# LayerNorm's output transposed by VectorE and DMA instead of TensorE, in a kernel of attention and an MLP

## The reference

```python
q_rot, k_rot = rotate(q), rotate(k)
scores = (1 / sqrt(64)) * q_rot @ k_rot.T
attn = exp(scores - max(scores)); attn = attn / (sum(attn) + 1e-9)
x = (attn @ v), heads side by side                  # 2304 x 512
h = x @ w_in                                        # 2304 x 1024
e = exp(h - max(h)); sm = e / (sum(e) + 1e-9)
solu = h * sm
ln = (solu - mean(solu)) / sqrt(var(solu) + 1e-6) * g_ln
out = ln @ w_out                                    # 2304 x 512
```

## Time and profile before

| | |
|---|---|
| Median of 3 runs | 521.86 us (521.09 to 523.84) |
| The profiled execution | 523.28 us, of which the span 521.5 us |
| TensorE busy | 495.7 us, 95% |
| VectorE busy | 341.9 us, 66% |
| ScalarE busy | 253.5 us, 49% |
| GpSimd busy | 117.3 us, 22% |
| DMA, mean | 84 GB/s; 27.7% of the 16 engines' time |
| Mean granted clock of TensorE | 0.993 |

### The profile page before, as it was taken

The page is one execution under the profiler, slowest core; times in us unless marked ns, Lnnn a source line. Parts: engine busy times, 40 slices in busy tenths (PEclk is TensorE's granted clock), DMA queues, the critical chain, the costliest instruction groups (busy, mean ns, idle before and its releaser), DMA issues.

```text
span 521.5 us, 7337 instructions
## 1 busy us (share of the span) xinstructions
PE 495.7 (95%) x2608; PEld 413.9 (79%) x2608; DVE 341.9 (66%) x554; ACT 253.5 (49%) x379; POOL 117.3 (22%) x84
## 2 busy tenths in 40 slices
PE   0799999989999999999999998999999999999997
PEld 0578888878888888888888876888888888888876
DVE  6957766776777677767774257967555666666550
ACT  3356776766677767776784341322222222222121
POOL 4701254235423542354321101001000000000000
PEclk9799999999999999999999999999999999999999
DMA  9115344534454545453612210010100000000001
GB/s 295 47 27 140 125 150 114 151 124 142 133 146 143 159 105 150 144 163 93 172 30 75 67 43 24 1 64 20 41 20 21 20 22 21 21 20 21 20 35 47
DMA packets 42789, 43.77 MB, mean 84 GB/s; under 512 B 31617, under 2 KB 31617, under 8 KB 40833
## 3 DMA queue, kind: packets, MB, share of 16 engines
q1 hardware_dynamic: 42728, 43.30, 27.7%
q10 hardware_dynamic: 24, 0.00, 0.0%
HBM read 33.63 MB, written 4.79 MB: 74 GB/s over the span
## 4 chain that ended last, share of the span: by engine, by line
PE 80%; issue 5%; SPq 5%; DMA 4%; DVE 3%; ACT 2%; ACTq 0%; POOL 0%; DVEq 0%; POOLq 0%
PE ps L831 19%; PE ps L858 18%; PE ps L844 17%; PE ps L800 14%; PE ps L773 7%; PE ps L868 3%; DMA w_raw<-w_in 3%; PE ps L813 2%; SPq L225 1%; DMA X<-x_in 1%; DVE nm L581 1%; SPq L216 1%; ACT p_main L434 1%; SPq L255 0%; SPq L254 0%
## 5 line engine op out<-in xcount | busy, mean ns | idle before, releaser
L581 DVE TENSOR_REDUCE nm<-ps 128x1 fp32r<-128x576 f32 x144 | 108.5, 756 | 74.9 <-PE ps L773 73.0
L831 PE MATMUL ps<-p_main,V 128*128 128x288 f32 x512 | 146.2, 409 | 0.0
L434 ACT ACTIVATE p_main<-ps 128x576 f32<-128x576 f32 x128 | 83.0, 648 | 52.8 <-PE ps L800 50.9
L800 PE MATMUL ps<-QK 128*128 128x288 f32 x320 | 97.4, 386 | 6.8 <-ACT p_main L434 3.7
L831 PEld LDWEIGHTS ps<-p_main,V 128*128 128x128 f32 x512 | 91.2, 192 | 14.3 <-ACT p_main L434 0.2
L858 PE MATMUL ps<-w_hi,QK 128*128 128x512 f32 x288 | 101.7, 421 | 0.0
L844 PE MATMUL ps<-w_hi,KB 128*128 128x512 f32 x288 | 92.8, 393 | 0.0
L773 PE MATMUL ps<-QK 128*128 128x288 f32 x320 | 68.8, 309 | 13.8 <-ACT QK L408 12.3
L800 PEld LDWEIGHTS ps<-QK 128*128 128x128 f32 x320 | 58.6, 192 | 27.6 <-ACT p_main L434 8.3
L317 POOL TENSOR_TENSOR X<-X,rope 128x1152 f32<-128x1152 f32 x14 | 37.1, 2653 | 141.3 <-DVE w_lo L598 112.0
L800 PE MATMUL ps<-KB 128*128 128x288 f32 x320 | 68.7, 297 | 0.0
(11 more groups left out here) (66 smaller groups left out, 523.8 us busy)
## 6 DMA issues: line engine op xcount, KB each, us to landing
X<-x_in SPq DMA_DIRECT2D x14, 1152.0 KB, 5.1
V<-v_in SPq DMA_DIRECT2D x32, 160.0 KB, 2.8
out<-X SPq DMA_DIRECT2D x18, 256.0 KB, 2.0
w_raw<-w_in SPq DMA_DIRECT2D x16, 256.0 KB, 3.0
xT<-oe SPq DMA_DIRECT2D x16, 144.0 KB, 2.4
inv<-inv_rows SPq DMA_DIRECT2D x16, 144.0 KB, 3.0
xT<-oe SPq DMA_DIRECT2D x16, 128.0 KB, 2.3
inv<-inv_rows SPq DMA_DIRECT2D x16, 128.0 KB, 3.0
```

What stands on the lines that cost most here:

```text
L434: nc.scalar.activation(dst[:, :].rearrange("p (b c) -> p b c", b=2), score_ps[:, :, 0:HALF], ACT.Exp, scale=SCALE).then_inc(exp_done, 1)
L581: nc.vector.tensor_reduce(nm[g][:, at:at + 1], src[:, :, 0:HALF], AX_XY, ALU.max, negate=True)\
L800: ins = nc.tensor.matmul(score_ps[:, half, 0:HALF], keys[:, of:of + P], queries[:, to + half * HALF:to + (half + 1) * HALF], start=(g == 0 ...
L831: ins = nc.tensor.matmul(o_ps[a][:, half, 0:HALF], v, p[:, half * HALF:(half + 1) * HALF], start=(k == 0), stop=(k == 9))
```

## The change

LayerNorm's output is no longer transposed by TensorE. VectorE transposes `ln` in 32 by 32 blocks in place (`turn_l`, one instruction of 128x1024), SP moves the 12 groups of blocks that belong to other partitions by DMA (`move_l`; each DMA has 32 partitions of 8 pieces of 128 bytes), GpSimd copies the 4 that stay (`stay`). `ln_high` and `ln_low` then read SBUF instead of PSUM. The buffers are the old `oe` and `V` of attention. The banks that are free so hold a third h; ups run four tiles ahead instead of three, with up(0) in steps 0 to 2 of the last pair, ups 1 to 3 after attention, and ups 16 and 17 back to back after down(12). SP issues move_l(t+3) after the store of tile t; moves 0, 1 and 2 stand between the last sums, output moves and inverses of attention.

At attention's start: the loads of pair 0 are merged into three; two memsets and the copies of the second queries of pair 0 go to GpSimd; TensorE multiplies the identity (24 times before the first row scores, once after each, 8 times before the first scores); the maxima of pair 1 are spread otherwise over the steps of pair 0, the first four in two PSUM slots. `w_raw` gets a second buffer. The order of the four parts of x in memory changes, so that one multiply by the table of cosines and sines serves keys and one queries.

```diff
-FIRST_MAXIMA = [[], [], [], [0], [1, 2], [3, 4], [5, 6], [7], [8]]
+FIRST_MAXIMA = [([], []), ([], []), ([], [0]), ([1], [2]), ([3], [4]), ([5], []), ([6], []), ([7], []), ([8], [])]
+SPARE = 4
+WARM_START, WARM_ROW, WARM_SCORE = 24, 1, 8
...
-        w_raw = sb("w_raw", [P, 512])
+        w_raw = [sb(f"w_raw{c}", [P, 512]) for c in range(2)]
...
-        h_ps = [ps[:, 0:2, :], ps[:, 2:4, :]]
-        t_ps = ps[:, 4:6, :]
+        h_ps = [ps[:, 0:2, :], ps[:, 2:4, :], ps[:, 4:6, :]]
+        turned_l = [oe[a][:, :, :].rearrange("p a s -> p (a s)")[:, 0:FF] for a in range(2)]
+        ln_T = [V[a][:, :, :, :].rearrange("p a b d -> p (a b d)")[:, 0:FF] for a in range(2)]
...
+        def blocks(l, group, k):
+            part = l[group * TURN:(group + 1) * TURN, :]
+            return part.rearrange("p (c k b) -> p c k b", k=GROUPS, b=TURN)[:, :, k, :]
+        def max_slot(k):
+            if k < STEPS:
+                return max_ps[k % 3], k - 2
+            if k < STEPS + SPARE:
+                return max_ps[2 * ((k - STEPS) % 2)], k - 1
+            return max_ps[0], k
+        def later(t):
+            last = TILES - 1 - AHEAD
+            return [] if t >= last else [t + AHEAD, t + AHEAD + 1] if t == last - 1 else [t + AHEAD]
...
+            def move_l(t):
+                a = t % 2
+                sp.wait_ge(l_turned, t + 1)
+                if t < 2:
+                    sp.wait_ge(pv_done, PVS * (PAIRS - 1 + t))
+                else:
+                    sp.wait_ge(l_lo_done, t - 1)
+                for of in range(GROUPS):
+                    for to in range(GROUPS):
+                        if of != to:
+                            sp.dma_start(blocks(ln_T[a], to, of), blocks(turned_l[a], of, to)).then_inc(l_moved[a], 16)
...
-            load_w(PAIRS - 1)
+            move_l(0)
             inverse_out(PAIRS - 2)
             sums(PAIRS - 1)
             move_o(PAIRS - 1)
             inverse_in(PAIRS - 2)
+            move_l(1)
             inverse_out(PAIRS - 1)
+            move_l(2)
             inverse_in(PAIRS - 1)
             for t in range(TILES):
                 sp.wait_ge(y_taken, t + 1)
                 sp.dma_start(out_d[t * P:(t + 1) * P, :], y[t % 2][:, :]).then_inc(stored[t % 2], 16)
+                if t + 3 < TILES:
+                    move_l(t + 3)
...
+            def first_second_queries(a):
+                at = COLS[a]
+                pool.wait_ge(rot_done, 1)
+                nc.gpsimd.tensor_copy(QK[0][other(a), 0, at:at + S], x_of(0)[own(a), 1, :]).then_inc(hi_done[a], 1)
...
+            def stay(t):
...
+                for group in range(GROUPS):
+                    nc.gpsimd.tensor_copy(blocks(ln_T[a], group, group), blocks(turned_l[a], group, group))\
+                      .then_inc(l_stayed, 1)
+                    pool.wait_ge(l_stayed, GROUPS * t + group + 1)
...
             for t in range(TILES):
                 power(t)
+                stay(t)
...
             def ln_high(t):
-                act.wait_ge(lnT_ready, t + 1)
-                nc.scalar.activation(l_hi[t % 2].rearrange("p (b c) -> p b c", b=2), t_ps, ACT.Copy)\
-                  .then_inc(l_hi_done, 1)
+                act.wait_ge(l_moved[t % 2], uses(t) * MOVES * 16)
+                act.wait_ge(l_stayed, GROUPS * (t + 1))
+                if t >= 2:
+                    act.wait_ge(y_ready, t - 1)
+                nc.scalar.activation(l_hi[t % 2], ln_T[t % 2], ACT.Copy).then_inc(l_hi_done, 1)
...
             take_o(PAIRS - 1, 1)
             w_high(PAIRS - 1)
+            add_eps(PAIRS - 1)
+            exp_h(1)
             ln_high(0)
-            exp_h(1)
-            add_eps(PAIRS - 1)
+            exp_h(2)
             for t in range(TILES):
                 if t + 3 < TILES:
-                    exp_h(t + 2)
-                if t + 3 == TILES - 1:
                     exp_h(t + 3)
...
+            def turn_l(t):
+                a, c = t % 2, (PAIRS - 2 + t) % 2
+                dve.wait_ge(ln_done, t * 2 + 2)
+                if t < 2:
+                    dve.wait_ge(sums_set[c], PAIRS // 2 * 32)
+                    dve.wait_ge(x_moved[c], PAIRS // 2 * 48)
+                else:
+                    dve.wait_ge(l_moved[a], uses(t - 2) * MOVES * 16)
+                    dve.wait_ge(l_stayed, GROUPS * (t - 1))
+                nc.vector.transpose(turned_l[a], ln[:, :]).then_inc(l_turned, 1)
...
             scale(0)
+            turn_l(0)
             invert(PAIRS - 2)
             w_low(PAIRS - 1)
-            ln_low(0)
             h_max(1)
             split_x(3)
             norm(1)
             scale(1)
+            invert(PAIRS - 1)
+            turn_l(1)
+            ln_low(0)
+            h_max(2)
+            split_x(4)
+            norm(2)
+            scale(2)
+            turn_l(2)
...
+            def keep_warm(count):
+                for _ in range(count):
+                    nc.tensor.matmul(score_ps[:, 0, 0:P], ident[:, :], ident[:, :], start=True, stop=True)
...
             for t in range(TILES):
-                if t + 3 == TILES - 1:
-                    for i in range(UPS):
-                        up(t + 3, i)
-                first = 16 if t == 0 else 4 if t + 3 < TILES else 0
                 for i in range(DOWNS):
                     down(t, i)
-                    if t + 1 < TILES and first <= i < first + FC:
-                        transpose_ln(t + 1, i - first)
-                if t + 3 < TILES - 1:
+                for tile in later(t):
                     for i in range(UPS):
-                        up(t + 3, i)
+                        up(tile, i)
```

More of the change, by code:

```diff
@@ L35 @@
 TURN = 32
+GROUPS = P // TURN
+MOVES = GROUPS * (GROUPS - 1)
 UPS = 6 * KC
 DOWNS = 3 * FC
+AHEAD = 4
 BOTH = 4
@@ L156, in attention_then_mlp @@
         ln_done = sem("ln_done")
-        lnT_ready = sem("lnT_ready")
+        l_turned = sem("l_turned")
+        l_moved = [sem(f"l_moved{a}") for a in range(2)]
+        l_stayed = sem("l_stayed")
         l_hi_done = sem("l_hi_done")
@@ L445, in w_high @@
             def w_high(m):
-                act.wait_ge(w_loaded, m * 16 + 16)
-                nc.scalar.activation(w_hi[:, m * 512:(m + 1) * 512], w_raw[:, :], ACT.Copy, scale=gain[:, m:m + 1])\
+                act.wait_ge(w_loaded[m % 2], uses(m) * 16)
+                nc.scalar.activation(w_hi[:, m * 512:(m + 1) * 512], w_raw[m % 2][:, :], ACT.Copy, scale=gain[:, m:m + 1])\
                   .then_inc(w_hi_done, 1)
@@ L686, in _ @@
                     add(2)
-                for i in maxima(0, s):
+                for i in maxima(0, s)[0]:
                     row_max(1, i)
@@ L690, in _ @@
                     low_keys(1, 1)
+                for i in maxima(0, s)[1]:
+                    row_max(1, i)
                 if s == 6:
@@ L699, in _ @@
                 for s in range(STEPS):
-                    for i in maxima(n, s):
+                    for i in maxima(n, s)[0]:
                         row_max(n + 1, i)
@@ L897, in _ @@
                             weigh(n, s)
-                    for i in maxima(n, s)[1:]:
+                    for i in maxima(n, s)[1]:
                         row_scores(n + 1, i)
```

194 lines of the change are left out of this document (91 added, 103 removed).

## The result

The changed kernel takes 517.98 us (median of four runs, 517.62 to 518.31) where the kernel before takes 521.91 in the runs beside it: a ratio of 0.992, 95% interval 0.989 to 0.995. That is 0.8% faster; 2.1% and 510.9 us were forecast. The sign was right and 518.0 lies in the range, but only 3.9 of the expected 11.0 us arrived.

What follows compares the result with a forecast made beforehand. TensorE, busy 95%, was taken to bound the kernel. up(1) at 302.5, plus 190.4 of blocks, 9.9 start, 4.6 end and 3.1 after the last matmul gave 510.5 us span, 510.9 median (2.1% faster); range 503 to 520.

Steps and rivals of the forecast that it cites:

- a sign of being wrong: Among the observations listed as showing the forecast wrong: GpSimd's copies of the staying blocks taking above 1 us.
- part 3: MLP's start: the new path is not yet ahead, so down(0) waits 5.1 us and down(1) 4.7.
- Part 4: MLP's end: down(15), down(16) and down(17) wait 1.0, 1.1 and 2.5 us for late moves and ln_low.
- the start costs 9.9 us: MLP's start: the waits of down(0) and down(1) on TensorE, added to the sum as 9.9 us.
- together 4.6 us: MLP's end: the waits of down(15) to down(17) on TensorE, added to the sum as 4.6 us.
- Part 2: New path's cost per tile: turn 1.24 us, 12 issues 7.6, landing 1.9, copies 1.6 to 3.6; steady period stays 10.88.
- Span to median: Whole kernel: the median of the runs stands 0.4 us above the profiled span, making 510.5 into 510.9 us.
- Part 5: Attention's ends and w_raw: gains of 2.0 us at the start, 2.2 from w_raw; sum 4.2 us.
- B: Rival: MLP's start and end hardly stall, SP issuing at 0.5 us; 504 to 507 us, floor 499; chance 0.17.
- C: Rival: slower, the SP queue becomes the bound, from 0.85 us per issue; 0.95 gives 541 us; chance 0.13.
- 335 + 216 s: SP queue as bound: total time in us, with s us per issue, 18 moves in line taking 216 s.
- D: Rival: VectorE becomes the bound, from turn plus collisions of 2.9 us; 529 us with 3.4; chance 0.05.

Runs made afterwards that it cites:

- e3_eps_behind: The changed kernel with add_eps(15) behind exp_h(1) on ScalarE instead of ahead of it: 513.16 us, ratio to before 0.984.
- e12_late_low: The changed kernel with ln_high(t+1) ahead of exp_h(t+3) on ScalarE, ln_low(t+2) right behind turn(t+3) and ln_low(1) behind turn(2) on VectorE: 513.64 us, ratio 0.983.
- e1_fill: The changed kernel with filler matmuls, results overwritten, before down(0), down(1), down(15), down(16) and down(17): 514.95 us, ratio to before 0.987.
- e8_dma16: The changed kernel with all 16 blocks moved by DMA from SP and none copied by GpSimd: 539.48 us, ratio to before 1.030.
- e4_one_w_raw: The changed kernel with one w_raw buffer and the loads of weights at their old places: 520.14 us, ratio to before 0.997.
- e5_order: e12_late_low with sums(15) and its output moves ahead of move(0) and an inverse on SP's queue: 509.12 us, ratio to before 0.974.
- e6_stay_act: The changed kernel with the four staying blocks copied by ScalarE ahead of ln_high instead of by GpSimd: 515.46 us, ratio to before 0.985.
- e10_split: e5_order with filler matmuls before down(16) and down(17), and the last tile's 12 moves split between SP's and ScalarE's queues: 504.75 us, ratio to before 0.968.
- e7_turn2: The changed kernel with VectorE turning each tile's output twice: 524.49 us, ratio to before 1.003.
- e2_no_warm: The changed kernel without the multiplications of the identity at attention's start: 520.0 us, ratio to before 0.996.

## Why the prediction missed

**Right.** The steady part: period 10.88, the turn 1.25 us (forecast 1.24, from the slope of other passes), twelve issues 7.8 to 7.9 us (7.6) and up to 8.8 where a slow one falls among them, landing 1.9 (1.9), stays 0.39 us at best and 0.40 in the median (0.4 to 0.9). One stay took 1.3 us, above the 1 us that was to be a sign of being wrong: it stood beside ln_low(0), whose subtract has both inputs in SBUF. ns min/median/max of the line:

```profile
L390 POOL COPY V<-oe x72: 387/396/1297, 304.0 to 495.2; 32x256 f32<-32x256 f32 x72
```

Also right was part 3's mechanism: the queue behind move(0), exp_h(1) behind add_eps(15), ln_low(1) behind tile 3; e3_eps_behind and e12_late_low took them away one by one. Waits there 4.4 and 4.6 (5.1 and 4.7); the 4.6 is in part luck, since down(1) started 1.2 us later from up(1) than forecast and the slow down(0) in front of it took 1.7 us out of its wait. Part 4: 0.9, 0.8 and 3.0 (1.0, 1.1, 2.5), by the steps named: take_y(13) at 484.7, store, move(16), store, move(17), all on SP. The chain at the end:

```profile
485.35 0.34 SPq L350
...
501.48 1.91 DMA V<-oe
503.42 1.06 ACT QK L531
504.51 1.24 DVE QK L692
505.74 0.04 issue
505.79 7.37 PE ps L940 x24
```

**The step that failed** is the price of a wait in parts 3 and 4, which stand at "the start costs 9.9 us" and "together 4.6 us". I charged the waits at their own length and every one of the 35 blocks at 5.44 us, as if a block took the same time behind a wait. The trace of before held the warning in the earlier trace rows: TensorE idle for 3 us, then half clock. (Its wait of 1.73 us was not followed by it.) I used it for attention's start, to credit the change with a gain, and did not apply it to waits of 3 to 5 us that I had just derived. Three blocks took 1.7 to 1.9 us more each; two of them are on the path, and e1_fill took 3.0 us off the median by mending them. Of the 7.1 us between forecast and median these 3.2 us are the largest term; 1.3 lie between span and median, 1.1 in collisions, 0.7 at up(1), and most of the rest is what a block took longer behind a wait at full clock (5.73 against 5.44). The mechanism (which downs wait, and for what) was right, the term was mis-sized.

**The collisions**, second. Part 2 charged nothing in the steady part, which holds because TensorE is the bound, though the cost is there: GpSimd's power lasts 1.4 us in place of 0.55, in the steady part (groups by line, 360 to 436 us; after, then e8_dma16, where ln_low runs at another moment):

```profile
L380 POOL TENSOR_TENSOR r<-r,expo 128x1 f32<-128x1 f32 x7 | 9.8, 1403 | 34.9 <-DVE r L715 34.9
```

```profile
L380 POOL TENSOR_TENSOR r<-r,expo 128x1 f32<-128x1 f32 x7 | 3.8, 550 | 73.7 <-DVE r L705 73.7
```

The subtract of ln_low, both of whose inputs are in SBUF now, beside one such power (VectorE and GpSimd in order of time, after):

```profile
340.06 1.22 DVE L692 TENSOR_TENSOR QK<-V,QK 128x1024 fp32r<-128x1024 f32 x1
341.72 0.16 DVE L719 TENSOR_TENSOR r<-r 128x1 f32<-128x1 f32 x1 [0.44 <-POOL r L380]
```

```profile
340.30 1.39 POOL L380 TENSOR_TENSOR r<-r,expo 128x1 f32<-128x1 f32 x1 [4.37 <-DVE r L715]
```

The power ends 0.4 us behind the subtract and VectorE waits 0.44 us for it, which is most of what VectorE's 9.8 us exceed the forecast 9.2 by (the 9.8 count this wait). By the rule that the prediction cited from the Trainium skill (SBUF - State Buffer, Who interferes with whom), a lock for a whole instruction, the power can't go on before the subtract has ended, and the trace agrees. Part 3 charged nothing either, and there VectorE is the path: split_x(4) took 1.2 us more beside GpSimd's last copy and its quotient, and down(1) started at 341.3 instead of 339.5, 0.7 of the 1.8 from up(1) and the rest of this size.

**Span to median**, third: +0.4 us forecast, +1.7 measured. The 0.4 presumed that the 1.4 us by which before's profiled execution stood above its median (523.3 and 521.9) were in the rows that the sum started from and would be in the other's too. The profiled execution of after stands 0.1 above its median, so the spans fell by 5.2 us and the medians by 3.9. Where the 1.4 us lay can't be told from one execution; among the executions here attention's start alone differs by 2.4 us.

**Part 5** came out in sum: w_raw 2.2 (2.2), attention's start 1.6 at pair 1 (2.0), the last pair 0.5 (0.8). But the half clock was not removed: it lies at 21.2 to 28.0 in the profiled execution, in those of e3_eps_behind, e4_one_w_raw, e5_order and e12_late_low at about 11.2 to 15.1, where exp(0,4) began at 30.4 to 30.9 instead of 31.8, and in those of e6_stay_act and e8_dma16 in two places (about 12 to 16 and 23 to 29), with exp(0,4) at 32.8 and 32.7. The start of attention is the same code in all of them, so this differs by execution. At this mark the changed kernel was even behind the kernel before (31.85 and 31.15 us); its 1.6 us are there only at pair 1.

**Rivals.** B's little stalling was within reach, but not for its reason: e5_order and e10_split lost most stalls through orders, fillers and a split, SP still issuing at 0.65, and e10_split's span of 502.4 us stands above B's floor of 499. C, the SP queue, did not bound the changed kernel, but it was nearer than "0.85 us per issue": e8_dma16 is worth 16/12 x 0.655 = 0.87 us per issue of twelve, the formula 335 + 216 s gives 524 for it, and its span was 539. The 335 counted 6 us for stores that take 18 x 0.65 = 11.7, and no long issues. With the 350 that fits this run the line meets the changed kernel's 516 at s = 0.77, not 0.85. D decides, with VectorE's 9.77 us, at 2.4 us for the turns alone, not at 2.9; e7_turn2 passed it with 2.5. Two bounds were worked out a little wrong, and nothing hung on them: the turn's upper one is 0.11 + 3.2 = 3.3 us, not 3.4, and half way from 0.53 to 1.83 us per issue is 1.2, not 1.0.

## What to carry to other kernels

A wait of some us on TensorE is priced with what follows it: read the clock of the stage behind each old wait of similar length, and count it only where no later wait swallows it. When an engine's step becomes many DMA issues, go through every entry of that queue at the start and the end of the loop and put what someone waits for in front of it; here one swap (e3_eps_behind, 4.8 us) gave more than the change itself (3.9). An order that helps the first tiles is to be walked through for the last ones too.

## What the runs showed of the hardware

- In the changed kernel TensorE's clock fell to its half level behind three of the five waits, which cost 1.6 us of 24 matmuls besides the wait; matmuls on ready operands in the wait prevented it (e1_fill). One of the three waits was 2.76 us; waits of 2.73 and 2.95 us in e6_stay_act and of 2.98 us at down(16) in e12_late_low were not followed by it.
- A DMA of 256 pieces of 128 bytes costs the issuing engine 0.65 us, and now and then 1.1 to 1.8; two engines issue at the same time at nearly full speed (0.64 and 0.70).
- A GpSimd instruction on one element per partition (128x1) took 1.40 us in place of 0.55 while VectorE subtracted two SBUF operands, a GpSimd copy of 32x256 1.30 in place of 0.40 beside the same, and a 128x1 multiply of VectorE 1.35 us in place of 0.16 beside a GpSimd multiply of 128x576.
- A profile can show the full clock where matmuls last as long as at half clock: 0.85 against 0.53 us for two matmuls of 288 columns at the start of e2_no_warm.
